# A blocked attention loop rewritten: mask by matmul, row sums from a ones column, logits inside the loop

## The chip, the cores and the metric

The kernel runs on one core of a Trainium2 chip, in one launch. Its time is the device time of one execution in microseconds (us). Engines: PE is TensorE, DVE is VectorE, ACT is ScalarE, POOL is GpSimd, SP is the sync engine, which here only issues DMAs. Of PE, weight loads (PEld) and matmuls are recorded apart.

## The reference, cut to what matters

```
# attention: B=2, H=8, S=768, D=64; block=32, window=16
k_sum = k.reshape(B, H, nb, block, D).max(axis=3)
v_sum = v.reshape(B, H, nb, block, D).mean(axis=3)
scores_l = where(|i - j| < window, scale * q @ k.T, -1e9)
scores_s = scale * q @ k_sum.T + log(block)
a = softmax over [scores_l, scores_s]          # max taken off, + 1e-9 in the sum
x = a @ [v, v_sum]                             # then reordered to (1536 tokens, 512)
# routing: 8 experts, 192 places each
logits = x @ w_gate
# the largest (token, expert) pairs are served first until an expert is full
out[mask_e] = relu(x[mask_e] @ w1[e]) @ w2[e]
# dense: h = x @ w_in; g = h if h >= 1, 0 if h <= -1, else (h+1)**2/4; g @ w_out
```

## The kernel before, in words

**Tiles.** Heads are taken two at a time: eight pairs t, one after the other. A query tile has 64 positions of each of the two heads, 128 rows in all; a pair has NT = 12 of them, worked on in NG = 3 groups g of GT = 4. G = 3t + g counts the 24 groups. A tile sees a window of 96 keys and 24 block maxima, KW = 120 columns. `q_diag` holds the queries with zeros beside them, so that one matmul scores both heads. `_nat` tiles are as loaded, two buffers u = t % 2.

**A pair's front (PE L818).** Six transposes of queries into `ps_q`, six of keys into `ps_k`. ACT copies the queries into `q_diag` (L770), DVE takes block maxima and fills `k_win` (`keys`, L701). The front of pair t+2 is the last thing that PE does in pair t (L879).

**A group.** PE: `turn` (transposes of the probabilities of group G), `scores` (of group G+2, into one of two PSUM buffers), `values` (of group G). The values matmul takes the 128 rows of both heads against the 128 value columns of both heads, of which the two diagonal 64x64 blocks are used. DVE (`mask_max`, L718): adds the mask while it moves the scores to SBUF as `masked`, takes the row maximum, negates and scales it. ACT (`exps`, L779): four exponentials with their row sums accumulated, and the copy of the transposed probabilities (`turned`). DVE (`out_rows`, L729): row sum + 1e-9, reciprocal, and four multiplies of 64x128 into `x_tok`, tokens by columns.

**The sync queue (L607).** Per pair t: wait until the keys of t are turned, load Q and K of t+2 (four DMAs), wait until the last values of t are done, load V of t+2 (eight DMAs), load the block means of t+2 from a DRAM scratch (two DMAs). POOL computes the block means in four parts from `v_blk` and stores them to the scratch (L637).

**The logit stage (L941 and around).** After all pairs: three stores of `x_tok` to `x_rows`; twelve rounds of four transposes of `x_tok`, an ACT copy, and a matmul with the gate weights as the stationary operand; a copy; twelve transposes; a DVE copy into `logit`. The routing chain of DVE, PE and ACT starts from `logit`. Experts and the dense part follow and are on PE.

Inside an engine everything runs in the order in which it is written; semaphores order the engines.

Of the kernel before, what the change touches and what calls it, by code (L numbers as in the profile page):

```python
# [16 lines left out]
P = 128  # L17
CREDIT = 8
# [11 lines left out]

def build(nc, q, k, v, w_gate, w1, w2, w_in, w_out, out):
# [17 lines left out]
    NEG = -1e9 / SCALE  # L49
    LOGB = float(np.log(BLOCK)) / SCALE  # L50
# [9 lines left out]
    vmean_dram = nc.dram_tensor("vmean_scratch", (B * H * NBLK, D), F32, kind="Internal").ap()  # L60
    vmean_pair = vmean_dram.rearrange("(t e n) d -> t n e d", e=2, n=NBLK)

    with ExitStack() as ctx:
# [429 lines left out]
        x_tok = token_ctx.enter_context(nc.sbuf_tensor("x_tok", [P, TT, DM], F32))  # L493


        with ExitStack() as actx:
# [5 lines left out]

            q_nat = [asb(f"q_nat{u}", [P, NTOK, 2 * D]) for u in range(2)]
            k_nat = [asb(f"k_nat{u}", [P, NTOK, 2 * D]) for u in range(2)]
            v_win = [asb(f"v_win{u}", [KW, NT, 2 * D]) for u in range(2)]
# [5 lines left out]
            mask = asb("mask", [P, NT, KW])  # L511
            thr_i = asb("thr_i", [P, NTHR])
            token_f = asb("token_f", [P, TT, 2])
            masked = [asb(f"masked{u}", [P, GT, KW]) for u in range(2)]
            row_max = asb("row_max", [P, 2, GT])
            neg_max = asb("neg_max", [P, 2, GT])
            prob = [asb(f"prob{u}", [P, GT, KW]) for u in range(2)]
            row_sum = asb("row_sum", [P, 2 * NG, GT])
            den = asb("den", [P, 2 * NG, GT])
            inv = asb("inv", [P, 2 * NG, GT])  # L520
            prob_t = [asb(f"prob_t{u}", [KW, GT, P]) for u in range(2)]

            ps_q = aps("ps_q", [P, 1024])
            ps_k = aps("ps_k", [P, 1024])
            ps_s = [aps(f"ps_s{u}", [P, GT, P]) for u in range(2)]
            ps_t = aps("ps_t", [P, GT, P])
            ps_o = aps("ps_o", [P, GT, P])

            s_q = [sem(f"s_q{u}") for u in range(2)]
            s_v = [sem(f"s_v{u}") for u in range(2)]  # L530
            s_vb = [sem(f"s_vb{g}") for g in range(VG)]
            s_vr = sem("s_vr")
            s_vm = sem("s_vm")
            s_mask = sem("s_mask")
            s_mk = sem("s_mk")
            s_zero = sem("s_zero")
# [3 lines left out]
            s_km = sem("s_km")  # L540
            s_kw = sem("s_kw")
            s_s = sem("s_s")
            s_ms = sem("s_ms")
            s_mx = sem("s_mx")
            s_nm = sem("s_nm")
            s_p = sem("s_p")
# [5 lines left out]
            s_x = sem("s_x")  # L552

            def pair_loop(eng, step):

                with eng.Fori(0, PAIRS // 2 - 1) as t2:
                    for u in range(2):
                        step(2 * t2 + u, t2, u)

            def all_steps(eng, step):  # L560

                pair_loop(eng, step)
                for u in range(2):
                    step(PAIRS - 2 + u, PAIRS // 2 - 1, u, to_come=1 - u)

            with nc.Block() as block:

                def load_qk(eng, t, u):
                    for e in range(2):
                        eng.dma_start(q_nat[u][:, :, e * D:(e + 1) * D],  # L570
                                     qp[t, e].rearrange("(n p) d -> p n d", p=P)).then_inc(s_q[u], 16)
                        eng.dma_start(k_nat[u][:, :, e * D:(e + 1) * D],
                                     kp[t, e].rearrange("(n p) d -> p n d", p=P)).then_inc(s_q[u], 16)

                @block.sync
                def _(sp):
                    def load_v(t, u):
                        lo, hi = TQ - WINDOW, S - WINDOW
                        for e in range(2):
                            c = slice(e * D, (e + 1) * D)  # L580
                            src = vp[t, e]
                            runs = src[lo:hi].rearrange("(j p) d -> p j d", p=TQ)
                            sp.dma_start(v_win[u][0:TQ, 1:NT, c], runs).then_inc(s_v[u], 16)
                            sp.dma_start(v_win[u][TQ:WIN, 0:NT - 1, c], runs[0:2 * WINDOW]).then_inc(s_v[u], 16)
                            sp.dma_start(v_win[u][WINDOW:TQ, 0, c], src[0:TQ - WINDOW]).then_inc(s_v[u], 16)
                            sp.dma_start(v_win[u][TQ:TQ + WINDOW, NT - 1, c], src[S - WINDOW:S]).then_inc(s_v[u], 16)

                    def load_means(t, u):
                        for e in range(2):
                            sp.dma_start(v_win[u][WIN:KW, :, e * D:(e + 1) * D],  # L590
                                         vmean_pair[t, :, e, :].unsqueeze(1).to_broadcast((NBLK, NT, D))
                                         ).then_inc(s_v[u], 16)

                    load_qk(sp, 0, 0)
                    sp.dma_start(wg[:, :, :], w_gate.rearrange("(k p) e -> p k e", p=P)).then_inc(s_wg, 16)
                    sp.dma_start(v_blk[:, 0, :], v_blocks[:, 0, :]).then_inc(s_vb[0], 16)
                    sp.wait_ge(s_zero, 4)
                    load_v(0, 0)
                    load_v(1, 1)
                    sp.dma_start(v_blk[:, 1, :], v_blocks[:, 1, :]).then_inc(s_vb[1], 16)  # L600
                    sp.wait_ge(s_vm, 16)
                    load_means(0, 0)
                    load_means(1, 1)
                    for g in range(2, VG):
# [10 lines left out]
                    pair_loop(sp, step)  # L615

                @block.gpsimd
                def _(pool):
                    pool.memset(ident[:, :], 0.0).then_inc(s_ident, 1)
                    pool.memset(mask[:, 0, 0:WIN], 0.0).then_inc(s_mask, 1)  # L620
# [5 lines left out]
                    pool.wait_ge(s_ident, 2)  # L626
                    done = 1
                    for sign, first in ((1, -1), (-1, 2 * WINDOW - 1)):
                        for e in range(2):
                            pool.wait_ge(s_mask, done)  # L630
                            m = mask[e * TQ:(e + 1) * TQ, 0, 0:WIN]
                            pool.affine_select(out=m, in_=m, compare_op=ALU.is_ge, fill=NEG, base=first,
                                               pattern=[[sign, WIN]], channel_multiplier=-sign).then_inc(s_mask, 1)
                            done += 1
                    pool.wait_ge(s_mask, done)

                    for part in range(VG):  # L637
                        pool.wait_ge(s_vb[part], 16)
                        width, done = BLOCK * D, 6 * part
                        while width > D:  # L640
                            width //= 2
                            pool.tensor_tensor(v_blk[:, part, 0:width], v_blk[:, part, 0:width],
                                               v_blk[:, part, width:2 * width], ALU.add).then_inc(s_vr, 1)
                            done += 1
                            pool.wait_ge(s_vr, done)
                        pool.tensor_scalar(v_mean[:, part, :], v_blk[:, part, 0:D], 1.0 / BLOCK, None,
                                           ALU.mult).then_inc(s_vr, 1)
                        pool.wait_ge(s_vr, done + 1)
                        if part:
                            pool.wait_ge(s_vm, 16 * part)  # L650
                        pool.dma_start(vmean_dram.rearrange("(g p) d -> p g d", p=4 * NBLK)[:, part, :],
                                       v_mean[:, part, :]).then_inc(s_vm, 16)
# [31 lines left out]
                def _(dve):  # L684
                    dve.sem_inc(s_x, CREDIT)
                    for u in range(2):
                        dve.memset(q_diag[u][:, :, :], 0.0).then_inc(s_zero, 1)
                    for u in range(2):
                        dve.memset(v_win[u][:, :, :], 0.0).then_inc(s_zero, 1)
                        dve.memset(k_win[u][:, 0, 0:WINDOW], 0.0)  # L690
                        dve.memset(k_win[u][:, NT - 1, WIN - WINDOW:WIN], 0.0)

                    dve.memset(mask[:, :, WIN:KW], LOGB).then_inc(s_mk, 1)
                    dve.wait_ge(s_mask, 5)
                    dve.tensor_copy(mask[:, 1:NT, 0:WIN],
                                    mask[:, 0:1, 0:WIN].to_broadcast((P, NT - 1, WIN))).then_inc(s_mk, 1)
                    dve.wait_ge(s_mk, 2)
                    dve.memset(mask[:, 0, 0:WINDOW], NEG).then_inc(s_mk, 1)
# [738 lines left out]
```

## Time and profile before

| | us |
|---|---|
| median of 3 runs | 708.82 (705.0 to 710.85) |
| the profiled execution | 713.24 |
| its span on the core | 711.5 |
| mean granted PE clock | 0.916 of full speed |
| busy: PE, PE weight loads, DVE, ACT, POOL | 620.8, 557.7, 401.9, 294.5, 56.7 |

The attention loop lies between 9 and 136 us, the logit stage reaches to 160 us, routing of the first two experts to about 222 us, experts and the dense part to the end. Times in the profile are us from the start of the span; a busy PE counts matmuls whose pipeline overlaps, so the spacing of starts tells more than the length of one.

### The profile page before, as it was taken

Reading aid. Unit: us, or ns where it says so; the run is one execution under the profiler, and the core shown is the slowest. Engines: PE = TensorE matmul, PEld = TensorE weight load, DVE = VectorE, ACT = ScalarE, POOL = GpSimd, SP = SyncE. Lnnn points to the kernel's source line nnn. Section 1 sums busy time; section 2 is a strip of 40 time slices with the busy share of each in tenths; the row PEclk is TensorE's granted clock in tenths of the full one; section 3 lists DMA queues with packets and bytes.
Section 4 is the critical chain, followed back from the end, with each engine's and each line's share of the span. In section 5 each row is a group of like instructions: output and inputs, shape, how many; then the busy total and the mean of one; then the engine's idle time right before and its main releaser. Section 6 shows DMA issues by size and latency. Waiting matters only on the chain.

```text
span 711.5 us, 13243 instructions
## 1 busy us (share of the span) xinstructions
PE 620.8 (87%) x4372; PEld 557.7 (78%) x4372; DVE 401.9 (56%) x1424; ACT 294.5 (41%) x720; POOL 56.7 (8%) x87
## 2 busy tenths in 40 slices
PE   2667787785549999999999998999999999999993
PEld 2667776433438999999999998999999989999992
DVE  6768878307774666666665015555555555555432
ACT  1545555333223234333242124454455454554441
POOL 3670000000101101011011000000000030000003
PEclk9879779695558999999999999999999999999998
DMA  9854561310612444445445555411112232000002
GB/s 182 188 115 101 109 129 42 115 64 1 222 37 83 164 155 148 169 153 186 158 159 180 197 187 146 142 60 60 60 64 82 88 142 69 3 0 1 1 1 89
DMA packets 95045, 75.58 MB, mean 106 GB/s; under 512 B 54624, under 2 KB 79264, under 8 KB 94624
## 3 DMA queue, kind: packets, MB, share of 16 engines
q1 hardware_dynamic: 89760, 67.94, 32.2%
q0 software_dynamic: 2112, 6.39, 2.6%
q10 hardware_dynamic: 3136, 0.79, 0.6%
q8 instruction: 20, 0.33, 0.2%
q14 instruction: 17, 0.14, 0.1%
HBM read 68.70 MB, written 6.40 MB: 106 GB/s over the span
## 4 chain that ended last, share of the span: by engine, by line
PE 62%; DVE 5%; issue 1%; ACT 1%; POOL 1%; DVEq 0%; ACTq 0%
PE ps_h L1327 10%; PE ps_o L1340 9%; PE ps_h L1303 6%; PE ps_o L1407 6%; PE ps_o L1409 6%; PE ps_o L1405 6%; PE ps_h L1305 6%; PE ps_h L1304 6%; PE ps_o L426 2%; DVE reach L244 1%; DVE mark L376 1%; PE ps_o L473 1%; POOL out L1292 1%; PE ps_o L444 0%; PE ps_o L1313 0%
## 5 line engine op out<-in xcount | busy, mean ns | idle before, releaser
L1327 PE MATMUL ps_h<-x_e,raw_a 128*128 128x192 f32 x512 | 102.8, 336 | 0.0
L1340 PE MATMUL ps_o<-h_e,raw_b 128*128 128x192 f32 x512 | 93.8, 327 | 0.0
L1303 PE MATMUL ps_h<-y_hi,a_hi 128*128 128x384 f32 x256 | 86.6, 338 | 2.3 <-DVE y_lo L1205 2.3
L1305 PE MATMUL ps_h<-y_hi,a_lo 128*128 128x384 f32 x256 | 86.7, 339 | 0.0
L1304 PE MATMUL ps_h<-y_lo,a_hi 128*128 128x384 f32 x256 | 86.4, 338 | 0.0
L395 ACT ACTIVATE reach<-thr,rest_half 128x256 bf16<-128x256 bf16 x132 | 56.3, 496 | 71.7 <-DVE rest_half L242 71.7
L1340 PEld LDWEIGHTS ps_o<-h_e,raw_b 128*128 128x128 f32 x512 | 84.6, 190 | 0.0
L1327 PEld LDWEIGHTS ps_h<-x_e,raw_a 128*128 128x128 f32 x512 | 82.3, 190 | 0.1
L1405 PE MATMUL ps_o<-b_hi,g_hi 128*128 128x512 f32 x192 | 74.9, 390 | 2.9 <-DVE g_lo L1264 1.7
L1409 PE MATMUL ps_o<-b_hi,g_lo 128*128 128x512 f32 x192 | 75.3, 392 | 0.0
L1407 PE MATMUL ps_o<-b_lo,g_hi 128*128 128x512 f32 x192 | 75.2, 392 | 0.0
L1264 DVE TENSOR_TENSOR g_lo<-g,g_hi 128x384 fp32r<-128x384 f32 x64 | 32.9, 554 | 72.6 <-ACT g_hi L1190 72.5
L1181 ACT ACTIVATE excess<-ps_h,minus 128x384 f32<-128x384 f32 x64 | 36.9, 577 | 66.6 <-DVE clip L1252 66.6
L1147 ACT ACTIVATE h_e<-ps_h 128x192 f32<-128x192 f32 x64 | 20.8, 324 | 97.6 <-PE ps_h L1327 97.6
L1190 ACT ACTIVATE g_hi<-g 128x384 fp32r<-128x384 f32 x64 | 30.1, 516 | 73.7 <-PE ps_o L1409 72.9
L784 ACT ACTIVATE prob<-masked,neg_max 128x120 f32<-128x120 f32 x96 | 36.7, 383 | 48.8 <-DVE neg_max L727 48.7
L859 PE MATMUL ps_o<-v_win,prob_t 120*128 120x128 f32 x192 | 32.6, 322 | 27.3 <-ACT prob_t L793 22.5
L244 DVE TENSOR_SCALAR reach<-thr,rest 128x256 bf16<-128x256 bf16 x264 | 54.5, 279 | 0.0
L859 PEld LDWEIGHTS ps_o<-v_win,prob_t 120*128 120x128 f32 x192 | 28.0, 224 | 31.1 <-ACT prob_t L793 24.2
L1303 PEld LDWEIGHTS ps_h<-y_hi,a_hi 128*128 128x128 f32 x256 | 48.6, 190 | 3.7 <-DVE y_lo L1205 2.5
L1304 PEld LDWEIGHTS ps_h<-y_lo,a_hi 128*128 128x128 f32 x256 | 48.5, 190 | 1.2
L1305 PEld LDWEIGHTS ps_h<-y_hi,a_lo 128*128 128x128 f32 x256 | 48.5, 189 | 0.0
(196 smaller groups left out, 986.7 us busy)
## 6 DMA issues: line engine op xcount, KB each, us to landing
raw_a<-in_moe_w SPq DMA_DIRECT2D x32, 512.0 KB, 3.5
raw_b<-in_moe_w SPq DMA_DIRECT2D x32, 512.0 KB, 4.8
raw_a<-in_moe_w_in SPq DMA_DIRECT2D x16, 512.0 KB, 3.4
raw_b<-in_moe_w_out SPq DMA_DIRECT2D x16, 512.0 KB, 5.1
v_blk<-in_v SPq DMA_DIRECT2D x4, 768.0 KB, 7.6
x_rows<-x_tok SPq DMA_DIRECT2D x3, 1024.0 KB, 6.9
v_win<-in_v SPq DMA_DIRECT2D x16, 176.0 KB
q_nat<-in_q SPq DMA_DIRECT2D x14, 192.0 KB, 3.3
```

The lines of the kernel that those rows point to most:

```text
L244: dve.tensor_scalar(reach[n][:, :], thr[:, table, :], src[:, n:n + 1], None, ALU.is_le).then_inc(s_reach, 1)
L395: act.activation(reach[n][:, :], thr[:, STEPS[s][0], :], ACT.Sign, bias=rest_half[:, n - TD:n - TD + 1], scale=-1.0).then_inc(s_sign, 1)
L859: ins = pe.matmul(ps_o[:, i, :], prob_t[w][:, i, :], v_win[u][:, GT * g + i, :], start=True, stop=True)
L1181: act.activation(excess[:, b, :], ps_h[:, b, 0:HC], ACT.Relu, bias=minus1[:, :]).then_inc(s_exc, 1)
L1303: pe.matmul(dst, hi_w, hi_x, start=first, stop=False, skip_group_check=True)
L1304: pe.matmul(dst, hi_w, lo_x, start=False, stop=False, skip_group_check=True)
L1305: return pe.matmul(dst, lo_w, hi_x, start=False, stop=last, skip_group_check=True)
L1327: ins = pe.matmul(ps_h[:, m % 2, 0:CAP], raw_a[r][:, kk, i * P:(i + 1) * P], x_e[:, kk, :], start=kk == 0, stop=kk == KT - 1)
L1340: ins = pe.matmul(ps_y[:, d, 0:CAP], raw_b[r][:, i, d * P:(d + 1) * P], h_e[m % 2][:, :], start=m == 0 and d % 2 == 0, stop=m == MU - 1, s ...
L1405: pe.matmul(ps_o2[:, t, :], g_hi[:, b, w], b_hi[s][:, :], start=m == 0, stop=False, skip_group_check=True)
L1407: pe.matmul(ps_o2[:, t, :], g_hi[:, b, w], b_lo[s][:, :], start=False, stop=False, skip_group_check=True)
L1409: ins = pe.matmul(ps_o2[:, t, :], g_lo[:, b, w], b_hi[s][:, :], start=False, stop=m == MU2 - 1, skip_group_check=True)
```

## The change

- **Mask.** Kept in bf16. `sel` and `mask` are multiplied in one matmul of 480 columns that opens the group's PSUM bank; the four score matmuls add to it. The queries carry the scale; log 32 is split into three bf16 parts. There are three score banks, so scores run three groups ahead.
- **Softmax.** DVE takes the negated maximum straight from PSUM; ACT reads PSUM too and accumulates no row sums.
- **Row sums and outputs.** `v_win` gets a column of ones per head (65 columns). Values are eight matmuls a group, one for each tile and head, 64 stationary columns by 65 moving ones, written to PSUM partitions 0 to 63 or 64 to 127, so that outputs stand by token. DVE then needs one multiply for the whole group.
- **Fronts.** Queries, keys and the turned columns of `x_tok` share one PSUM tile `ps_f`. Keys of pair t+2 are turned after group 0 of pair t, queries after group 1, columns of pair t-1 after group 2.
- **Logits.** Per pair six transposes of `x_tok` (`turn_columns`), an ACT copy (`columns`), six matmuls of 8 columns (`logits`), which add up in PSUM over the pairs. The logit stage is gone; DVE copies `logit` at the end of the loop.
- **Queues.** The SP queue now loads K, then Q, then V and means of t+2, then waits for the outputs of pair t and stores their columns to `x_rows`. Means come from `v_mean` in SBUF; the scratch is gone. DVE computes part 0 of the block means, POOL the others. The first K load and the first `v_blk` go by ACT's queue. SP loads the three other `v_blk` parts before its loop.
- The loops over pairs are written out instead of being run by registers.

```diff
-                    def step(t, t2, u):
-                        sp.wait_ge(s_tk, t + 1)
-                        load_qk(sp, t + 2, u)
-                        sp.wait_ge(s_o, CREDIT + NG * t + NG)
-                        load_v(t + 2, u)
-                        sp.wait_ge(s_vm, 16 * t2 + 32)
-                        load_means(t + 2, u)
+                    load_q(sp, 0, 0)
+                    load_q(sp, 1, 1)
+                    load_k(sp, 1, 1)
+                    sp.wait_ge(s_zv, 6)
+                    load_v(0, 0)
+                    load_means(0, 0)
+                    load_v(1, 1)
+                    load_means(1, 1)
+                    sp.dma_start(wg[:, :, :], w_gate.rearrange("(k p) e -> p k e", p=P)).then_inc(s_wg, 16)
+                    for g in range(1, VG):
                         sp.dma_start(v_blk[:, g, :], v_blocks[:, g, :]).then_inc(s_vb[g], 16)
+                    for t in range(PAIRS):
+                        if t + 2 < PAIRS:
+                            sp.wait_ge(s_tk, t + 1)
+                            load_k(sp, t + 2, t % 2)
+                            sp.wait_ge(s_tq, t + 1)
+                            load_q(sp, t + 2, t % 2)
+                            sp.wait_ge(s_o, NG * t + NG)
+                            load_v(t + 2, t % 2)
+                            load_means(t + 2, t % 2)
+                        sp.wait_ge(s_x, NG * t + NG)
+                        rows = slice(t // HP * NTOK, (t // HP + 1) * NTOK)
+                        sp.dma_start(x_cols[t % HP][:, rows, :],
+                                     x_tok[:, rows, t % HP * 2 * D:(t % HP + 1) * 2 * D]).then_inc(s_xs, 16)
...
+                    def row_max(G):
                         dve.wait_ge(s_s, G + 1)
+                        if G >= 3:
+                            dve.wait_ge(s_pr, G - 2)
+                        dve.tensor_reduce(neg_max[:, G % 3, :], score_tiles(G), AX.X, ALU.max,
+                                          negate=True).then_inc(s_nm, 1)
+
+                    def out_rows(G):
+                        t, g = divmod(G, NG)
+                        dve.wait_ge(s_o, G + 1)
+                        dve.tensor_scalar(den[:, :, :], o_sum[:, :, :, D], 1e-9, None, ALU.add).then_inc(s_dn, 1)
                         dve.wait_ge(s_dn, G + 1)
+                        dve.reciprocal(inv[:, :, :], den[:, :, :]).then_inc(s_iv, 1)
                         dve.wait_ge(s_iv, G + 1)
...
+                        dve.tensor_tensor(x_tok[:, row:row + GN, cols].rearrange("p n (e d) -> p n e d", e=2),
+                                          o_sum[:, :, :, 0:D],
+                                          inv[:, :, :].unsqueeze(3).to_broadcast((P, GN, 2, D)),
+                                          ALU.mult).then_inc(s_x, 1)
...
+                    def exps(G):
                         act.wait_ge(s_nm, G + 1)
...
                         for i in range(GT):
+                            ins = act.activation(prob[G % 2][:, i, :], tiles[:, i, :], ACT.Exp,
+                                                 bias=neg_max[:, G % 3, i:i + 1])
+                        ins.then_inc(s_pr, 1)
...
+                    def turn_columns(t):
+                        pe.wait_ge(s_x, NG * t + NG)
+                        row, col = t // HP * NTOK, t % HP * 2 * D
+                        for n in range(NTOK):
+                            ins = pe.transpose(ps_f[:, n * P:(n + 1) * P], x_tok[:, row + n, col:col + 2 * D],
+                                               ident[:, :])
+                        ins.then_inc(s_xt, 1)
+
+                    def logits(t):
+                        pe.wait_ge(s_xc, t + 1)
+                        for n in range(NTOK):
+                            ins = pe.matmul(logit_sum[:, t // HP * NTOK + n, :], x_t[t % 2][:, n * P:(n + 1) * P],
+                                            wg[:, t % HP, :], start=t == 0 and n == 0, stop=t % HP == HP - 1,
+                                            skip_group_check=True)
+                        ins.then_inc(s_lg, 1)
...
+                        tiles = score_tiles(G)
+                        pe.matmul(tiles, sel[:, :], mask[:, GT * g:GT * g + GT, :], start=True, stop=False,
+                                  skip_group_check=True)
                         for i in range(GT):
                             j = GT * g + i
+                            ins = pe.matmul(tiles[:, i, :], q_diag[u][:, j, :], k_win[u][:, j, :],
+                                            start=False, stop=True, skip_group_check=True)
...
+                        for n in range(GN):
+                            for e in range(2):
+                                for par in range(2):
+                                    i = 2 * n + par
+                                    ins = pe.matmul(o_sum[par * TQ:(par + 1) * TQ, n, e, :],
+                                                    prob_t[G % 2][:, i, e * TQ:(e + 1) * TQ],
+                                                    v_win[u][:, GT * g + i, e, :], start=True, stop=True)
...
+                    for G in range(GROUPS_A):
+                        t, g = divmod(G, NG)
+                        turn(G)
+                        if G + 3 < GROUPS_A:
+                            scores(G + 3)
+                        values(G)
+                        if g == 0:
+                            if t >= 2:
+                                logits(t - 2)
+                            if t + 2 < PAIRS:
+                                if t >= 2:
+                                    pe.wait_ge(s_xc, t - 1)
+                                else:
+                                    pe.wait_ge(s_kr if t == 0 else s_qd, t + 2)
+                                turn_keys(t + 2, t % 2)
+                        if g == 1 and t + 2 < PAIRS:
+                            pe.wait_ge(s_kr, t + 3)
+                            turn_queries(t + 2, t % 2)
+                        if g == 2 and t >= 1:
+                            if t + 2 < PAIRS:
+                                pe.wait_ge(s_qd, t + 3)
+                            else:
+                                pe.wait_ge(s_xc, t - 1)
+                            turn_columns(t - 1)
+                    logits(PAIRS - 2)
+                    turn_columns(PAIRS - 1)
+                    logits(PAIRS - 1)
```

## Rows read from the trace of the kernel before

**Rows 1.** Stretches: busy us (instructions) of each engine, PE clock, DMA share, GB/s.
```profile
90.00:120.00 30.00, 22.85 (x157) 21.69 (x157) 25.34 (x76) 18.08 (x68) 0.00 (x0) 0.84 0.46 99
...
240.00:700.00 460.00, 453.29 (x3124) 419.00 (x3123) 245.77 (x831) 196.11 (x416) 16.89 (x19) 1.00 0.31 105
```

**Rows 2.** Waits, 30 to 125 us: waiter, releaser, total us, times, longest.
```profile
ACT prob L784 <- DVE neg_max L727: 38.2, 20, 2.9
```

**Rows 3.** Timeline, one group of four tiles at full clock, key transposes, small last transposes.
```profile
96.24 0.69 PEld L829 LDWEIGHTS ps_k<-ident,k_nat 128*128 128x128 f32 x6
...
104.57 0.66 DVE L722 TENSOR_TENSOR masked<-ps_s,mask 128x480 f32<-128x480 f32 x1
...
105.26 0.65 DVE L725 TENSOR_REDUCE row_max<-masked 128x4 f32<-128x480 f32 x1
...
105.61 0.47 PEld L849 LDWEIGHTS ps_t<-ident,prob 128*120 128x120 f32 x4
...
106.06 0.97 PEld L840 LDWEIGHTS ps_s<-k_win,q_diag 128*128 128x128 f32 x8
...
106.73 1.20 DVE L742 TENSOR_TENSOR x_tok<-ps_o,inv 64x128 f32 x4 [0.33 <-DVE inv L734]
...
107.96 0.66 DVE L722 TENSOR_TENSOR masked<-ps_s,mask 128x480 f32<-128x480 f32 x1
...
108.31 0.97 PEld L859 LDWEIGHTS ps_o<-v_win,prob_t 120*128 120x128 f32 x8 [1.28 <-ACT prob_t L793]
...
158.69 0.83 PEld L964 LDWEIGHTS ps_l<-ident,logit_t 8*128 8x128 f32 x12 [2.46 <-ACT logit_t L936]
```

**Rows 4.** Timeline, the sync queue's V loads, and values ahead of them.
```profile
14.17 0.60 SPq L583 DMA_DIRECT2D v_win<-in_v  x1
...
16.46 0.60 SPq L583 DMA_DIRECT2D v_win<-in_v  x1
...
54.34 0.65 SPq L583 DMA_DIRECT2D v_win<-in_v  x1
...
94.79 1.06 PE L859 MATMUL ps_o<-v_win,prob_t 120*128 120x128 f32 x8
...
96.02 0.63 SPq L583 DMA_DIRECT2D v_win<-in_v  x1
...
102.17 0.39 SPq L570 DMA_DIRECT2D q_nat<-in_q  x1
...
109.64 0.63 SPq L583 DMA_DIRECT2D v_win<-in_v  x1
```

**Rows 5.** K load's landing after its issue starts; the stores' issue.
```profile
DMA to landing us min/median/max: 3.0/3.3/3.5
...
135.96 2.10 SPq L912 DMA_DIRECT2D x_rows<-x_tok  x3
```

**Rows 6.** PE after its longest wait in the loop; the clock behind it.
```profile
39.87 1.54 PE L824 MATMUL ps_q<-ident,q_nat 128*128 128x128 f32 x6 [4.11 <-DMA k_nat<-in_k]
...
41.00:43.00 2.00, 2.00 (x11) 2.00 (x11) 0.27 (x1) 1.54 (x2) 1.89 (x2) 0.50 0.59 132
43.00:45.00 2.00, 2.00 (x18) 1.94 (x17) 2.00 (x5) 0.67 (x2) 1.71 (x4) 0.97 0.79 181
```

**Rows 7.** Timeline of the start: first masking, block loads, blocked issue.
```profile
18.62 0.66 DVE L722 TENSOR_TENSOR masked<-ps_s,mask 128x480 f32<-128x480 f32 x1 [2.22 <-PE ps_s L840]
...
26.15 0.86 SPq L605 DMA_DIRECT2D v_blk<-in_v  x2
...
30.45 4.54 SPq L572 DMA_DIRECT2D k_nat<-in_k  x1
...
35.92 0.64 SPq L583 DMA_DIRECT2D v_win<-in_v  x1
```

**Rows 8.** Timeline of the logit stage: last outputs, logit copy.
```profile
134.49 1.20 DVE L742 TENSOR_TENSOR x_tok<-ps_o,inv 64x128 f32<-64x128 f32 x4 [2.00 <-PE ps_o L859]
...
159.71 0.26 DVE L220 COPY logit<-ps_l 128x96 f32<-128x96 f32 x1 [24.03 <-PE ps_l L964]
```

More of the change, by code:

```diff
@@ L28, in shapes, with bf16_parts @@
     return c
+def bf16_parts(value, count):
+    parts = []
+    for _ in range(count):
+        part = float((np.array([value], np.float32).view(np.uint32) & np.uint32(0xFFFF0000)).view(np.float32)[0])
+        parts.append(part)
+        value -= part
+    return parts
 def build(nc, q, k, v, w_gate, w1, w2, w_in, w_out, out):
@@ L615, in _ @@
-                    pair_loop(sp, step)
+                            part, row = divmod(2 * t + e, 4)
+                            if part == 0:
+                                sp.wait_ge(s_vr0, MEAN_ADDS + 1)
+                            else:
+                                sp.wait_ge(s_vr, (MEAN_ADDS + 1) * part)
+                            rows = v_mean[row * NBLK:(row + 1) * NBLK, part, :]
+                            sp.dma_start(v_win[u][WIN:KW, :, e, 0:D],
+                                         rows.unsqueeze(1).to_broadcast((NBLK, NT, D))).then_inc(s_v[u], 16)
@@ L635, in _ @@
[L635 to L643, printed above, removed]
+                    pool.wait_ge(s_mask, 3)
@@ new lines, in _ @@
+                    pool.wait_ge(s_mask, 6)
+                    pool.affine_select(out=band, in_=band, compare_op=ALU.is_ge, fill=NEG, base=2 * WINDOW - 1,
+                                       pattern=[[-1, WIN]], channel_multiplier=1).then_inc(s_mask, 1)
+                    for i, part in enumerate(LOGB_PARTS):
+                        if i:
+                            pool.wait_ge(s_mask, 7 + i)
+                        pool.affine_select(out=blocks, in_=blocks, compare_op=ALU.not_equal, fill=part, base=-i,
+                                           pattern=[[0, NBLK]], channel_multiplier=1).then_inc(s_mask, 1)
@@ L644, in _ @@
+                    pool.wait_ge(s_mask, 7 + len(LOGB_PARTS))
+                    pool.memset(q_diag[1][:, :, :], 0.0).then_inc(s_zq[1], 1)
+                    done = 0
+                    for part in range(1, VG):
+                        for n in block_means(pool, part, s_vr):
                             done += 1
                             pool.wait_ge(s_vr, done)
-                        pool.tensor_scalar(v_mean[:, part, :], v_blk[:, part, 0:D], 1.0 / BLOCK, None,
-                                           ALU.mult).then_inc(s_vr, 1)
@@ new lines, in _ @@
+                    keys(0, 0)
+                    row_max(0)
+                    row_max(1)
+                    row_max(2)
+                    done = 0
+                    for n in block_means(dve, 0, s_vr0):
+                        done += 1
+                        dve.wait_ge(s_vr0, done)
+                    keys(1, 1)
+                    for G in range(GROUPS_A):
+                        t, g = divmod(G, NG)
+                        if G + 3 < GROUPS_A:
+                            row_max(G + 3)
+                        out_rows(G)
+                        if g == 0 and t + 2 < PAIRS:
+                            keys(t + 2, t % 2)
@@ L812, in _ @@
-                    all_steps(act, step)
+                    for G in range(GROUPS_A):
+                        t, g = divmod(G, NG)
+                        turned(G)
+                        if G + 2 < GROUPS_A:
+                            exps(G + 2)
+                        if g == 1 and t + 2 < PAIRS:
+                            queries(t + 2, t % 2)
+                        if g == 2 and t >= 1:
+                            columns(t - 1)
+                    columns(PAIRS - 1)
                 @block.tensor
@@ L861, in values @@
                         ins.then_inc(s_o, 1)
                     pe.wait_ge(s_ident, 2)
-                    front(0, 0, 0)
-                    scores(0, 0, 0, 0, 0)
-                    scores(1, 0, 1, 0, 1)
-                    front(1, 0, 1)
-                    def step(t, t2, u, to_come=2):
-                        for g in range(NG):
-                            G = NG * t + g
-                            w = (u + g) % 2
-                            turn(G, w)
-                            if g + 2 < NG:
-                                scores(G + 2, t, g + 2, u, w)
-                            elif to_come:
-                                scores(G + 2, t + 1, g + 2 - NG, 1 - u, w)
-                            values(G, t2, g, u, w)
-                            if g == NG - 1 and to_come == 2:
-                                front(t + 2, t2 + 1, u)
@@ L882, in _ @@
-                    all_steps(pe, step)
-        s_xt = sem("s_xt")
-        s_xc = sem("s_xc")
-        s_xu = sem("s_xu")
-        s_ltc = sem("s_ltc")
-        s_lg = sem("s_lg")
+                    turn_queries(0, 0)
+                    pe.wait_ge(s_qd, 1)
+                    turn_keys(0, 0)
+                    pe.wait_ge(s_zk, 4)
+                    pe.wait_ge(s_mk, 3)
+                    for G in range(3):
+                        scores(G)
+                    pe.wait_ge(s_kr, 1)
+                    turn_queries(1, 1)
@@ L909, in _ @@
                 def _(sp):
-                    for c in range(NCH):
-                        tiles = slice(c * CH, (c + 1) * CH)
-                        sp.dma_start(x_dram.rearrange("(n p) d -> p n d", p=P)[:, tiles, :],
-                                     x_tok[:, tiles, :]).then_inc(s_xs, 16)
                     sp.wait_ge(s_sel, 1)
```

356 lines of the change are left out of this document (146 added, 210 removed).

## The prediction, made before the changed kernel was timed

> **What bounds the kernel now.** I read the stretch table first, then the waits inside the loop, then one group of tiles, one pair on the sync queue, the start, and the logit stage. Only the first 160 us are touched: from 240 to 700 us PE is busy 453 of 460 us at full clock [rows 1], and nothing there is edited. In 90 to 120 us DVE is busy 25.3 of 30 us, PE 22.9 at a mean clock of 0.84. In the loop ACT waits for DVE's maxima, 38 us in 20 waits [rows 2], and PE in turn for ACT: DVE sets the pace. One group of four tiles repeats every 3.39 us (104.57 to 107.96) [rows 3]: masking 0.66, maximum 0.65, negation, denominator and reciprocal, outputs 1.20. With the keys a pair takes 13.6 us: V loads start at 96.02 and again at 109.64; from 54.34 on, four pairs took 55.3 us, 13.8 each [rows 4]. The sync queue is beside all this: it needs 6.15 us (96.02 to 102.17) for the ten loads of V and means and still idles before the next pair, because its Q and K are needed only at the end of the following pair.
>
> **Part by part: engines of the loop.** DVE loses the masking (0.66), the negation (0.17, a small step) and most of the outputs: one 128x256 instruction of about 0.4 us (between the 0.30 of one 64x128 and the 0.66 of 128x480) for four of 1.20 [rows 3]. What stays is 0.65 + 0.4 + about 0.7 for denominator, reciprocal and their gaps, 1.8 us a group. Keys stay, 2.9 us a pair. So DVE would need 8.3 us a pair and stops being the bound. ACT loses four accumulator reads a group and gains one 128x768 copy a pair, 0.8 us; it was idle 38 us of 95 in one wait alone [rows 2], so it is at nothing, covered by PE.
>
> PE gains. By weight loads issued back to back at full clock [rows 3]: transposes 0.47, scores 0.97, values now 0.97 for 8 passes of 128 columns. The values become 16 passes of 65 columns with 64-column weights. Bounds: 16 x 0.069 = 1.1, by the row of the small transposes (12 in 0.83), or half a pass if they scale, 0.97; above, 16 x 0.12 = 1.9. I take 1.0, as half-size operands stand nearest to half a pass. The mask matmul (bf16, 480 columns) has no such row; between a score tile (0.24) and two of them (0.5) above and nothing below; I take 0.2. A group is 2.65 us. Keys and queries 0.69 each, columns 0.69, logits 12 x 0.069 = 0.85 (above 1.5). A pair of PE work at full clock: 3 x 2.65 + 2.07 + 0.85 = 10.9 us, with gaps 11.5. That would gain 2 us a pair, if the data were there.
>
> **The load of the keys.** It is not, and this is the term that decides. PE turns the keys of pair t+2 right after the first group of pair t. The sync queue issues their load only at its step t, behind step t-1: the ten loads of V and means for t+1, which wait for the last values of pair t-1, and then the new store of the columns of t-1. Call the end of those values T (before, 94.79 + 1.06 = 95.85). The queue wakes 0.17 later [rows 4]. Eight V loads: in straight code at the start four take 16.46 - 14.17 = 2.29, so 4.6; means 0.84; together 5.4 (6.15 as in the loop before is the upper bound, 4.7 the lower, issue times without gaps). Store: 0.7 (three in 2.10 [rows 5]; its wait, x_tok of that pair, ends while V is issued). First K load 0.5; the second lands 3.3 after it starts [rows 5]. Sum: T + 10.1, 10.2 with PE's wake. PE comes there at T + 2.65 + 0.85 (logits) + 0.7 (columns of the pair before) = T + 4.2, and stands 6 us. All that is behind it in its queue waits: turning group 3t+1, its scores, its values. DVE and ACT run three and two groups ahead, then stand too. And the loop closes on itself: V loads of the next pair wait for the values that wait for these keys, so nothing is caught up.
>
> After the stall PE has, up to the next T: keys 0.69, group 2.65, queries 0.69, group 2.65 = 6.7 at full clock, and some 0.3 of latency. Clock: after 4.1 us without work PE came back at 39.87 at level 0.50 (1.2 GHz) and was full again only after 43 us [rows 6]. So I take 4.5 us at half clock, which does 2.25 of the work: 4.5 + 4.4 + 0.3 = 9.2. Bounds: 7.0 (full), 13.7 (half all through). DVE's keys (2.9) lie beside group 3t+1 and are no later than its values. Period 10.2 + 9.2 = **19.4 us against 13.8** (16.7 to 24).
>
> **The start.** The values of pair 0 end at 35.7 before (the queue's wake follows at 35.92 [rows 7]). After: the first scores come a little earlier than the 18.62 of before [rows 7], though the one PSUM buffer for queries and keys puts two copies in series; three score groups at half clock bring the third maximum to 21 us; the block means of part 0 on DVE (1984 elements, 480 in 0.65, plus six waits) 2.7, so 24; then means 0.8, V of pair 1 4.6, means 0.8, three v_blk: about 31. The K load of pair 2 stands behind these three blocks. Before, two blocks and four Q/K loads, 2.3 MB, issued from 26.15, had landed at 39.87, 13.7 us, with 4.54 us in one blocked issue [rows 6, 7]. Now 2.7 MB must pass from about 29: 12 to 16 us, so 43 (41 to 46). Then 9.2: pair 0's values end at 52 (49 to 56), 16 later than before. The loads in front also push the means of pair 0, which come at 27 to 28, in time for its first values.
>
> **The end and the logit stage.** Pairs 6 and 7 turn no keys: 11.3, and 10.6 without scores. Then, after the last outputs, columns, copy, logits, copy for two pairs: 2 x (0.7 + 0.2 + 0.9 + 0.2) + 0.9 + about 1.5 of the remaining queueing = 6.4. Before, from the end of the last outputs (134.49 + 1.20) to the logit copy at 159.71 were 24.0 us [rows 8]. So the removed stage gives back 18 us. The later x_rows stores, the constants on GpSimd and wg cost nothing: they are needed near 190 us.
>
> **Sum.** 52 + 5 x 19.4 + 11.3 + 10.6 + 6.4 = 177.3 us for the logit copy, against 159.7: +17.6. The profiled execution took 713.2 (span 711.5); 730.8. It lies 4.4 above the median of the three runs, 708.8, so **726 us**.
>
> **A rule beside it.** The values' two halves write PSUM partitions 0 to 63 and 64 to 127 in turn. No row of before has such a pair. The Trainium skill (TensorE: Matmul & The Clock Gate, Part 3) says that matmuls whose outputs lie in different column groups run concurrently; no run shown has tested it here. See rival three for what it would be worth.
>
> **Rivals.**
> 1. *The keys come in time (faster).* If issue and landing were hidden, the loop would run at PE's 11.5 to 12: 52 + 60 + 28.3 = 140.3, -19.4, median **689**. For: the queue idles before its V loads now, and 768 packets are little. Against: the wait for the last values stands in the chain whatever the speed. It decides once the keys land less than 6.6 us after T: a pair then takes 15.9, and 52 + 5 x 15.9 + 28.3 is the 159.7 of before; the chain of rows gives 10.1. Chance 0.19.
> 2. *Stall, but short, and the start cheap (no change):* period 17, pair 0's values done at 48: 48 + 85 + 28.3 = 161.3, +1.6, **710**. For: lower bounds of issue and clock. Chance 0.13.
> 3. *Halves of the values overlap:* a group is 0.5 cheaper, two in a period, six in the last pairs: -5 -3, **718**. Chance 0.10. By the rule named above this is the case to expect, at the same stall.
> 4. *Small passes cost as much as large:* 16 x 0.12, +0.95 a group: +9.5 +5.5, **741**. For: no row shows a 64-column weight load, so a floor is open. Chance 0.13, with half clock throughout (period 24, 749) as its far end.
> 5. *My forecast,* 19.4 a period: 0.45.
>
> **How the numbers follow.** Faster by over 1% (under 701.7): rival 1 and a little of 2, 0.2. Within 1%: 0.13. Slower: the rest, 0.67; 1% is about what these runs, which spread by 0.8%, can tell. Range: my case with periods 17.5 to 22 and the start's bounds reaches 713 to 742; taking in rival 2 and the short end, **703 to 742**, which leaves out rival 1 and the far end of 4.
>
> **What would show it.** V loads of successive pairs in the sync queue 19 us apart; PE's longest total wait in 50 to 150 us on k_nat's load, five times near 6 us, clock 0.50 behind each; the first at 30 to 43 us. Group of values 1.0 at full clock or less (rival 3) or 1.9 (rival 4). Logit copy near 177, and 6 us behind the last x_tok. I am wrong if the keys' load is issued less than 4 us after the V loads begin, or if PE waits for DVE or ACT instead.

## The result, and the profile after

| | before | after |
|---|---|---|
| median on the chip of the prediction, 4 runs each | 707.54 (705.0 to 710.85) | 738.35 (737.57 to 738.99) |
| the profiled execution, its span | 713.24, 711.5 | 738.28, 736.5 |
| logit copy, end of the changed part | 159.71 | 184.34 |
| from there to the end of the span | 551.8 | 552.2 |

The change made the kernel slower: ratio 1.0432, 95% interval 1.0384 to 1.048. 726 was forecast, in 703 to 742; the measured 738.35 lies inside, 12 us above the point forecast and 4 below the upper bound. What the profiles differ by lies ahead of the logit copy, but for 0.4 us.

Stretches of the changed kernel, with the columns of [rows 1]; the second line answers to its second, and is as busy as that.

```profile
90.00:120.00 30.00, 20.75 (x212) 19.11 (x211) 11.83 (x33) 13.94 (x36) 0.00 (x0) 0.80 0.34 74
...
250.00:725.00 475.00, 468.32 (x3302) 433.20 (x3299) 256.69 (x891) 200.98 (x429) 16.99 (x19) 1.00 0.32 106
```

DVE, busy 25.3 of 30 us before, has 11.8 left, and no engine has become the bound: PE is busy 20.8. Waits up to 190 us, with the columns of [rows 2]:

```profile
PE ps_f L866 <- DMA k_nat<-in_k: 47.9, 6, 9.6
...
ACT prob L819 <- DVE neg_max L757: 7.7, 2, 7.4
```

ACT's wait for the maxima is down from 38.2 us in 20 waits [rows 2] to 7.7 in two; PE now waits for the load of the keys, six times, 48 us in all. One pair on the sync queue and on PE, answering to [rows 4, 5]:

```profile
136.94 0.69 PE L922 MATMUL ps_o<-v_win,prob_t 120*64 120x65 f32 x16 [0.81 <-ACT prob_t L827]
137.56 0.88 PE L873 MATMUL ps_f<-ident,x_tok 128*128 128x128 f32 x6
137.67 0.68 SPq L610 DMA_DIRECT2D v_win<-in_v  x1
...
139.89 0.69 PE L922 MATMUL ps_o<-v_win,prob_t 120*64 120x65 f32 x16
...
140.50 1.50 PE L880 MATMUL ps_l<-wg,x_t 128*128 128x8 f32 x12
...
142.37 1.74 SPq L624 DMA_DIRECT2D v_win<-v_mean  x2
144.16 0.53 SPq L650 DMA_DIRECT2D x_rows<-x_tok  x1
144.74 1.49 SPq L588 DMA_DIRECT2D k_nat<-in_k  x2
...
149.47 1.51 PE L866 MATMUL ps_f<-ident,k_nat 128*128 128x128 f32 x6 [7.46 <-DMA k_nat<-in_k]
...
158.17 0.68 SPq L610 DMA_DIRECT2D v_win<-in_v  x1
```

The chain reads down the rows: values end at 137.6 (136.94 + 0.69), V loads from 137.67, means 142.37, store 144.16, keys 144.74, landed 149.47, next pair's V loads at 158.17. PE has done group, columns and logits by 142.0 and stands 7.5 us. The clock behind such a wait, answering to [rows 6]:

```profile
150.00:152.00 2.00, 2.00 (x10) 1.90 (x9) 0.98 (x2) 0.13 (x1) 0.00 (x0) 0.50 0.11 17
152.00:154.00 2.00, 2.00 (x21) 1.86 (x21) 1.89 (x6) 1.48 (x5) 0.00 (x0) 0.68 0.00 0
154.00:156.00 2.00, 2.00 (x27) 1.91 (x22) 1.12 (x4) 0.84 (x2) 0.00 (x0) 1.00 0.00 0
```

And the start, answering to [rows 7]: PE stands twice, first for the gate weights (the profile names no releaser; the next section shows it), then for pair 2's keys.

```profile
33.06 1.08 PE L907 MATMUL ps_t<-ident,prob 128*120 128x128 f32 x4 [11.08 <-issue]
...
45.64 1.51 PE L866 MATMUL ps_f<-ident,k_nat 128*128 128x128 f32 x6 [8.34 <-DMA k_nat<-in_k]
...
54.24 0.69 PE L922 MATMUL ps_o<-v_win,prob_t 120*64 120x65 f32 x16 [0.81 <-ACT prob_t L827]
```

### The profile page after: what moved, and what is told of

It is laid out like the page before. It is cut to its first block, busy times and chain, and to the rows that moved or that the text cites. A ratio compares the mean times of both kernels' runs of the same rounds, so it can differ in the third digit from the quotient of the medians.

```text
span 736.5 us, 13215 instructions
## 1 busy us (share of the span) xinstructions
PE 613.0 (83%) x4648; PEld 558.8 (76%) x4648; DVE 363.6 (49%) x1316; ACT 279.5 (38%) x620; POOL 50.8 (7%) x80
## 4 chain that ended last, share of the span: by engine, by line
PE 60%; DVE 4%; issue 1%; ACT 1%; POOL 1%; DVEq 0%; ACTq 0%
PE ps_h L1360 10%; PE ps_o L1373 9%; PE ps_o L1440 6%; PE ps_o L1442 6%; PE ps_o L1438 6%; PE ps_h L1336 6%; PE ps_h L1338 6%; PE ps_h L1337 6%; PE ps_o L433 2%; DVE mark L383 1%; DVE reach L251 1%; PE ps_o L480 1%; POOL out L1325 1%; PE ps_o L451 0%; PE ps_h L1397 0%
## 5 line engine op out<-in xcount | busy, mean ns | idle before, releaser
L1180 ACT ACTIVATE h_e<-ps_h 128x192 f32<-128x192 f32 x64 | 20.8, 325 | 99.1 <-PE ps_h L1360 99.1
L866 PE MATMUL ps_f<-ident,k_nat 128*128 128x128 f32 x48 | 11.5, 406 | 51.4 <-DMA k_nat<-in_k 47.9
L866 PEld LDWEIGHTS ps_f<-ident,k_nat 128*128 128x128 f32 x48 | 8.6, 210 | 52.6 <-issue 48.4
L827 ACT ACTIVATE prob_t<-ps_t 120x512 f32<-120x512 f32 x24 | 14.3, 596 | 87.9 <-PE ps_t L907 87.8
## 6 DMA issues: line engine op xcount, KB each, us to landing
v_win<-in_v SPq DMA_DIRECT2D x16, 176.0 KB
```

## The experiments

They ran on four chips, each kernel beside the kernel before on the same chip (medians of the kernel before 719.3 for e1 to e3, 705.9 for e4, e5, e6 and the repeat of the change, 717.8 for e7, 721.4 for e8). So times are compared as ratios to before, and traces by the logit copy. Where one run was made, that is said. Theory A is that of the prediction: the keys' load, issued behind V, means and store, closes a loop of about 20 us.

**e1, Q and K one pair earlier.** The buffers are free then, so nothing but the order of the queue changes. The first four lines, for pair 2, stand behind the v_blk loads:

```diff
+                    sp.wait_ge(s_tk, 1)
+                    load_k(sp, 2, 0)
+                    sp.wait_ge(s_tq, 1)
+                    load_q(sp, 2, 0)
                     for t in range(PAIRS):
+                        if t + 3 < PAIRS:
+                            sp.wait_ge(s_tk, t + 2)
+                            load_k(sp, t + 3, (t + 1) % 2)
+                            sp.wait_ge(s_tq, t + 2)
+                            load_q(sp, t + 3, (t + 1) % 2)
                         if t + 2 < PAIRS:
-                            sp.wait_ge(s_tk, t + 1)
-                            load_k(sp, t + 2, t % 2)
-                            sp.wait_ge(s_tq, t + 1)
-                            load_q(sp, t + 2, t % 2)
                             sp.wait_ge(s_o, NG * t + NG)
```

> The changed kernel with Q and K loaded one pair earlier: step t of the sync queue issues those of pair t+3 before it waits for pair t's last values; those of pair 2 stay behind the three v_blk loads. Theory A (the load of the keys, issued behind V, means and store, closes the loop at 20.6 us a pair): the wait for k_nat goes from all pairs but the first, V loads of successive pairs stand 11 to 13 us apart, five periods give back 38 to 48 us: 690 to 700 us. Theory B (the keys' wait only covers waits of PE for ACT and DVE, which take its place): period 17 or more, time above 720. The wait before pair 2's keys, near 10 us, stays under both.

Measured: 701.36, ratio 0.9758 (0.9722 to 0.9794). V loads of the sync queue, and PE's turning of the keys of pairs 3 and 7, in its timeline:

```profile
55.20 0.68 SPq L610 DMA_DIRECT2D v_win<-in_v  x1
...
57.38 0.87 PE L871 MATMUL ps_f<-ident,k_nat 128*128 128x128 f32 x6
...
65.26 0.74 SPq L610 DMA_DIRECT2D v_win<-in_v  x1
...
76.11 1.61 SPq L610 DMA_DIRECT2D v_win<-in_v  x1
...
103.22 0.85 PE L871 MATMUL ps_f<-ident,k_nat 128*128 128x128 f32 x6
...
110.47 0.67 SPq L610 DMA_DIRECT2D v_win<-in_v  x1
```

From 55.20 to 110.47 a pair takes 11.05 us instead of 20.64, in the mean of five; the first are cheaper, and from pair 3 on, by the keys' rows, it is a steady 11.46. The only wait for keys left is the first, 8.1 us at pair 2. The order of one queue turns 4.3% slower into 2.4% faster; theory B falls.

**e2, pair 2's Q and K ahead at the start too** (the four lines for pair 2 moved ahead of the first means).

> As the run with Q and K one pair earlier, and those of pair 2 issued right after pair 0's V, ahead of the means and of the three v_blk loads. Theory A: pair 0's values end near 36 to 40 us instead of 54.8, so 15 to 19 us less than the other: 673 to 683 us. Theory C (the start is bound by the block means and V of pair 1, not by the keys of pair 2): less than 5 us from the other.

Measured: 693.26, ratio 0.9653 (0.9611 to 0.9695), and 0.9671 (0.9635 to 0.9707) on the chip of e8. Pair 0's values end at 44.8, 10 us earlier and not 15 to 19, and the time is 8.1 us below e1: neither theory's forecast, A's of 15 to 19 or C's of under 5, was met. Its timeline shows what stands there:

```profile
31.04 0.54 SPq L639 DMA_DIRECT2D wg<-in_moe_w_gate  x1
...
33.41 1.08 PE L912 MATMUL ps_t<-ident,prob 128*120 128x128 f32 x4 [11.28 <-issue]
...
34.41 10.08 SPq L583 DMA_DIRECT2D q_nat<-in_q  x2
```

PE waits ahead of its first group for the gate weights, which it needs only two pairs later, and two issues behind the three v_blk loads take 10.1 us. In the changed kernel the wait for pair 2's keys stood behind both and hid them.

**e3, a dose of issue time.**

```diff
                             load_means(t + 2, t % 2)
+                            for i in range(6):
+                                sp.dma_start(idle[:, 6 * t + i, :], vp[t, 0][S - WINDOW:S]).then_inc(s_idle, 16)
```

> The changed kernel with six more loads of 16 rows of 256 bytes a pair, to a tile of their own, issued between the means and the store; 0.42 us of issue each and next to no data. Theory A: the keys come 3.0 us later in each of five periods, V loads 23.6 us apart instead of 20.6, time +15: 753. Theory B: period unchanged within 1 us, 738 to 743.

Measured in one run: V loads at 54.87 and 173.37, 23.70 us a pair, 3.06 more; 764.3 us, where 753 was forecast. The logit copy is 18.2 us later than in the changed kernel (202.54), and the part behind it takes 560.1 us on this chip instead of 552.2; the two make up the 26 us between 738.35 and 764.3. The waits from 50 to 180 us and the added issues:

```profile
PE ps_f L870 <- DMA k_nat<-in_k: 54.7, 5, 12.6
```

```profile
84.88 2.84 SPq L651 DMA_DIRECT2D idle<-in_v  x6
```

Six issues, 2.84 us in all, come back as 3.06 us a pair, at 24 KB of data. It is the queue's issue time that is on the path. (The changed kernel had no run on this chip, so 764.3 has no direct partner.)

**before_again, a second profile of the kernel before.**

> The kernel before, unchanged, for a second profile: its profiled execution took 713.2 us while its median is 707.5. If the 5 us lie in the start (loads that land late, the wait of 4.1 us at 39.87), the values of pair 0 still end near 35.7 and the later pairs' V loads come earlier; if they are spread, the clock's level differs in the routing or the loop.

Measured: 717.7 on a chip where its median is 719.3; logit copy at 151.22, 8.5 us earlier than in the profile that the prediction used, with the first V loads after pair 0 at 38.96 and 52.36 and pairs of 13.5 us. What is left from the copy to the end takes 564.7 us here and 551.8 there. So the part that was edited differs by 8.5 us between two profiles of the same kernel, on two chips, and the part behind it by 13. The pairs differ little; 5.4 of the 8.5 us lie behind the last V loads (109.64 and 106.51). There the windows show the clock, the profile of the prediction first:

```profile
124.00:136.00 12.00, 6.62 (x33) 5.67 (x33) 6.77 (x25) 4.25 (x17) 0.00 (x0) 0.68 0.00 1
```

```profile
120.00:130.00 10.00, 5.20 (x41) 4.40 (x39) 6.75 (x24) 4.16 (x17) 0.00 (x0) 1.00 0.00 1
```

In the logit stage it was 0.87 (136 to 160 us) against 1.00 (130 to 151.3). PE's long wait for a load was one of 3.8 us for the means ahead of 27.36 here, where it was one of 4.1 for keys at 39.87.

**after_again.**

> The changed kernel, unchanged, on the chip of these runs: V loads 20.6 us apart, logit copy at 184 to 185, and the part behind it as long here as in the other kernels of this chip. If the part behind differs by 8 us between chips, 745; otherwise 738.

Measured in one run: 736.8 (before 705.9 there, ratio 1.044), 20.43 us a pair (54.76 to 156.91), copy at 183.21, 551.9 behind it. The slowdown repeats.

**e4, the start mended.** Two edits on e2:

```diff
                     load_means(1, 1)
+                    sp.wait_ge(s_tk, 2)
+                    load_k(sp, 3, 1)
+                    sp.wait_ge(s_tq, 2)
+                    load_q(sp, 3, 1)
...
-                    pe.wait_ge(s_wg, 16)
...
                     def logits(t):
+                        if t == 0:
+                            pe.wait_ge(s_wg, 16)
```

> As the run with Q and K early at the start too, with two edits: PE waits for the gate weights ahead of the first logits, not ahead of the first group (in the other run it stood 11.3 us there, until 33.4), and Q and K of pair 3 are loaded ahead of the three v_blk loads. Theory: pair 0's values end at 35 to 38 us instead of 44.8, the loop stays at 10.4 to 11.5 us a pair, logit copy at 117 to 121 instead of 126.5; 6 to 10 us less than the other, ratio to before 0.952 to 0.958. Rival: v_blk's parts, needed for the means of pair 2, or V of pair 1 take the wait over and less than 3 us are won.

Measured: 681.94, ratio 0.9641 (0.957 to 0.9712); again 0.9609 (0.9572 to 0.9646) on e7's chip. Pair 0's values end at 36.6, as the theory said, so the wait of 11 us was for the gate weights. But the time did not follow: the ratio is that of e2 within the intervals, not 0.952 to 0.958, and the logit copy stands at 130.36 (e2: 126.51 and 129.63). The rival took it over.

```profile
35.67 1.69 SPq L645 DMA_DIRECT2D v_blk<-in_v  x3
...
39.02 4.98 SPq L612 DMA_DIRECT2D v_win<-in_v  x1
```

```profile
53.88 1.13 PE L933 MATMUL ps_o<-v_win,prob_t 120*64 120x65 f32 x16 [5.47 <-DMA v_win<-v_mean]
```

V of pair 2 stands behind three blocks of 768 KB, its means are issued at 50.5, and PE waits 5.5 us for them. The queue's order is not the only candidate for that wait. From 36 to 50 us the DMA share is 1.13, so the DMA engines were full too. And POOL, which makes the means of pair 2 from the first of the three blocks, is done with them only at 49.1 (48.73 + 0.40), so they could not have been issued before.

**e5, the values' matmuls by half.** `for par in range(2)` is moved from the innermost loop of `values` to the outermost; same 16 passes.

> As e4, with the 8 matmuls of a group's values in another order: four into PSUM partitions 0 to 63, then four into 64 to 127, instead of in turn. If the 0.55 us for 16 passes come from neighbours in different column groups running at once, the passes take 0.8 to 1.0 us, PE-bound pairs 11.8 to 12.4, time 6 to 10 us above e4. If they come from the operands' size alone: 0.55 as before, same time.

Measured: 687.1 in one run, 4 us above e4's profiled 683.2 (e4's runs spread by 2.7), the logit copy 2.8 later. Weight loads of one group, e4 first, then e5:

```profile
69.35 0.55 PEld L933 LDWEIGHTS ps_o<-v_win,prob_t 120*64 120x64 f32 x16
```

```profile
68.33 0.83 PEld L933 LDWEIGHTS ps_o<-v_win,prob_t 120*64 120x64 f32 x16
```

In turn a pass costs 34 ns, grouped 52 ns, against 121 ns for one of 128x128 [rows 3]. Both are at work: size more than halves a pass, and neighbours in different column groups take off another third. By 24 groups that is 6.7 us, by three groups a pair 0.84; a pair bound by PE takes 12.02 us instead of 11.46 (11.8 to 12.4 forecast), so two thirds come through. The time, forecast 6 to 10 us longer, is 4 to 5 longer.

**e6, columns and logits of all pairs behind the loop** (the same calls, after it, on PE and ACT).

> As e4, with the turning of the columns and the logits of all eight pairs behind the loop instead of in it (same instructions). In the loop they cost PE 0.64 + 1.41 a pair where PE is the bound: pairs at 9.0 to 9.8 instead of 11.05. Behind it, a chain of turn 0.65, copy 0.9, next turn, with 1.41 of logits beside it: 2.2 to 2.6 a pair, 18 to 21 us. Sum: 5 to 9 us slower than e4 (6 us of tail fall away, 19 come, 10 to 13 are won in the loop). If PE is not the bound in the loop, 12 us or more slower.

Measured: 692.65, ratio 0.9782 (0.9684 to 0.988), 10.7 us above e4 by the medians, between the two forecasts; its four runs lie at 688 and at 697, so 6 to 15 is what can be said. In the loop the pairs came at 10.2 to 11.7 us, not 9.0 to 9.8. The queue needs 10 us a pair (V 4.7, means 1.75, store 0.55, K 1.5, Q 1.4), and PE waits for keys again, 6.9 us in four waits: the load is the next bound. Behind the loop a pair took 3.73 us, not 2.2 to 2.6, at half clock (0.50 from 115 to 120 us):

```profile
116.11 2.57 PE L890 MATMUL ps_l<-wg,x_t 128*128 128x8 f32 x12
118.53 1.52 PE L881 MATMUL ps_f<-ident,x_tok 128*128 128x128 f32 x6
119.84 2.57 PE L890 MATMUL ps_l<-wg,x_t 128*128 128x8 f32 x12
```

Columns and logits inside the loop are worth some 11 us; the logits cost 1.5 a pair there, at full clock, the columns 0.64.

**e7, v_blk loads apart.** Part 1 behind V of pair 1, parts 2 and 3 at the ends of steps 0 and 1 of the queue.

> As e4, with the three v_blk loads apart: part 1 behind V of pair 1, part 2 at the end of the queue's step 0, part 3 at the end of step 1. In e4 the three in a row blocked the queue (one V load of 4.98 us, V and means of pair 2 done only at 52), and PE waited 5.5 us for means at pair 2. Theory (the queue behind three blocks of 768 KB is what is left of the start): that wait is gone, pairs 10.4 to 11.3 us from the first, logit copy at 119 to 124 instead of 130.4, 6 to 11 us less than e4: 671 to 676, ratio to before 0.945 to 0.957. Rival (the block means themselves or the K load of pair 3, now behind part 1, come late): less than 3 us won.

Measured: 690.28, ratio 0.9612 (0.9578 to 0.9646); e4 beside it 0.9609. The theory falls in this form. PE's wait for means shrank to 0.6 us, and waits for keys took its place:

```profile
56.46 1.51 PE L879 MATMUL ps_f<-ident,k_nat 128*128 128x128 f32 x6 [3.70 <-DMA k_nat<-in_k]
...
70.61 1.51 PE L879 MATMUL ps_f<-ident,k_nat 128*128 128x128 f32 x6 [1.08 <-DMA k_nat<-in_k]
```

Keys issued behind a block landed 6.4 to 7.5 us after their issue, against 3.6 to 4.1 in the changed kernel, and from 48.9 to 56.5 us the DMA share is 1.06. At each place tried in that queue, the load behind a block is late; whether the queue's order or the full DMA engines do it, e7 does not tell.

**e8, v_blk on POOL's queue,** each part when POOL has done with the one before:

```diff
-                    for g in range(1, VG):
-                        sp.dma_start(v_blk[:, g, :], v_blocks[:, g, :]).then_inc(s_vb[g], 16)
...
                     for part in range(1, VG):
+                        pool.dma_start(v_blk[:, part, :], v_blocks[:, part, :]).then_inc(s_vb[part], 16)
```

> As e4, with the three later v_blk parts loaded by POOL's own queue, each when POOL has done with the part before, so that they stand in no other load's way. Theory (what is left of the start is the sync queue standing behind 768 KB blocks): no wait of PE for V, means or K after 30 us longer than 1 us, no issue on the sync queue over 3 us; V loads 10.4 to 11.5 us apart from the first; logit copy at 118 to 124; ratio to before 0.945 to 0.955. Rival (the DMA engines are simply full in this stretch, whoever issues): waits of 3 to 6 us for K or means stay, ratio 0.957 to 0.965.

Measured: 686.82, **ratio 0.9527** (0.9493 to 0.9561), the lowest ratio of all kernels tried; e2 took 696.7 on the same chip. Logit copy at 123.49. PE from 39.7 to 95 us, with the columns of [rows 1]:

```profile
39.70:95.00 55.30, 49.57 (x568) 45.79 (x568) 33.32 (x90) 34.90 (x90) 9.66 (x26) 1.00 0.77 164
```

From 25 us to the last pair no row of the sync queue is over 2.7 us, and V loads come 11.4 to 11.8 us apart, the last two 8.9 apart. PE waits for a load once, 2.2 us for the means at 30.37, which misses the forecast of no wait over 1 us; in the stretch above it waits for none. So the three blocks that e4 loads at 35.67 were what was left of the start. That it is the queue and not the DMA engines is not shown, for the edit also moves the loads in time:

```profile
22.95 0.58 POOL L688 DMA_DIRECT2D v_blk<-in_v  x1 [0.31 <-POOL v_mean L599]
...
35.66 0.55 POOL L688 DMA_DIRECT2D v_blk<-in_v  x1 [0.29 <-POOL v_mean L599]
```

With the first at 4.9, two of the three blocks are issued before 23 us, where e4 issues all three behind 35.67. POOL has the means of pair 2 at 22.6 instead of 49.1, and from 36 to 50 us the DMA share is 0.78 (177 GB/s) instead of 1.13 (224). A run with the blocks as early, but on the sync queue, would part the two; there is none. The Trainium skill (Trainium Kernel Development and Optimization, Key Constraints) says that several issuing engines share the same 16 DMA engines and that this "only saves the sequencer's issue time". What e8 gains beyond issue time no run here separates; that issue time of the sync queue can be the path, e3 shows.

## Why the prediction was right, and where its sizes were off

**The deciding term held.** The load of the keys, chained behind the V loads of the pair before, was put at a period of 19.4 us with a wait of 6; measured 20.64 and 7.4 to 9.6. e1 removes it by order alone, e3 scales it: 2.84 us of issues gave 3.06. Term by term, from 137.6 to 158.1: wake 0.04 (0.17 forecast), V 4.70 (4.6), means 1.79 (0.84), store 0.58 (0.7), keys from issue to PE 4.73 (3.8 and 0.1), PE's work 8.7 (9.2). The mis-sized ones are the means, whose issue from SBUF costs 0.87 us each where that from DRAM cost 0.42, and the landing of the keys, 3.6 to 4.1 us where [rows 5] had a median of 3.3. Why it is longer was not tried; these loads stand behind a store of 384 KB, and where e4 issued keys with no store ahead, at 32.6, they landed in 3.1 to 3.4.

**The start.** Pair 0's values end at 54.9, forecast 52 (49 to 56). The keys' wait ended at 45.6 for 43. But the step by which wg, the gate weights, "cost nothing: they are needed near 190 us" failed: I had read the stage that used them before, not the wait that the change puts ahead of the first group. It cost 11 us of standing, hidden behind the keys, so the sum did not show it; e2 and e4 did.

**The end.** From the last V loads' T, 158.1, to the logit copy 26.2 us, forecast 28.3. The last outputs are done at 176.0, the copy follows 8.3 later where I had 6.4: the two last logits ran at or near half clock (2.45 and 2.73 us for 1.50; granted clock 0.57 from 176 to 184 us), and had been priced too low.

**PE's prices.** Mask matmul and scores came at 0.10 + 1.06 by weight loads (1.17 forecast), transposes 0.47 (0.47). Logits took 1.41, not 0.85: the row of 8x128 weights was the wrong neighbour for 128x128 weights, and the upper bound of 1.5 was near. Values took 0.55 for 1.0. Rival 3, the rule of column groups, was right in its mechanism and nearly in its size (0.45 less a group), as e5 shows: 0.28 of the 0.45 is that rule, the other 0.17 the size of the operands, where I had taken half a pass. The stall hides it in one group of three, as rival 3 reckoned; in the two others it is part of why PE's work came at 8.7 for 9.2. Rival 4 is out. Rival 1 was wrong as a forecast, but e1 and e8 show that its engine side was right: freed of the stall, PE is the bound, with no wait for a load, at 11.46 to 11.48 us a pair by the keys' rows, forecast 11.5. That agreement is partly luck: the weight loads of a pair add up to 9.9 us where I had 10.9, and the gaps between them to 1.6 where I had 0.6.

**The sum.** Logit copy +24.6 us where +17.6 was forecast: +2.9 start, +6.2 for five periods, -2.1 end. The medians moved by 30.8. The other 6 us are from the step "it lies 4.4 above the median": the profiled execution of before stood 5.7 above the median in the end, while that of after is at its median, so the excess should have been taken off the edited part, not carried over. before_again, with its copy at 151, shows that this part of the kernel before does vary by that much, and that more than half of it lies where the clock was 0.68 and 0.87 instead of 1.00; why the clock was lower there is open. That 738 still fell inside the range owes something to its upper end, which stood for a longer period and not for this.

## What to carry to other kernels

When work on an engine is moved forward in a pair's order, move its load forward in the queue's order too, and write out the queue as a chain: what each issue waits for, the issue times in front, the landing, and who closes the loop. A wait that stands in front of another hides it; after mending one, read the start again. Large loads that nobody needs soon should not stand ahead of urgent ones: e8, which issued them on another queue and earlier, has its logit copy 7 us before e4's.

## What the runs showed that was not expected

- One of the two issues of block means a pair costs 0.87 us from SBUF and 0.42 from DRAM, for the same 288 runs of 256 bytes.
- Passes of 120x64 weights by 65 columns in f32: 34 ns in turn over the two column groups, 52 ns grouped, 118 ns for 128x128 weights by 8 columns.
- The part of the program that nobody edited takes 551 to 552 us in the profiles of the result and of e4 to e6 and the repeat of the change, and 557 to 565 on the three other chips, in every kernel run there; only ratios to before on the same chip can be compared.
